# Down projection of 18 half experts in seven block products instead of eight, in a kernel of retention and two mixture-of-experts layers

## The reference

```python
# layer 1: N, D, E, F = 1536, 512, 8, 1024; layer 2: the same with E = 4
for e in range(E):
    h = np.maximum(x @ w1[e], 0.0)        # [1536, 1024]
    ye = h @ w2[e]                        # [1536, 512]
    out += P[:, e:e + 1] * ye
```

## Time and profile before

| | us |
|---|---|
| median of 3 runs | 1545.9 (1545.72 to 1546.02) |
| profiled execution, first to last instruction (span) | 1544.1 |
| profiled execution, own time | not listed apart from the span |
| TensorE busy | 1538.1 (100%) |
| VectorE busy | 880.1 (57%) |
| ScalarE busy | 446.9 (29%) |
| GpSimd busy | 49.5 (3%) |

### The profile page before, as it was taken

The page is one execution under the profiler, slowest core; times in us unless marked ns, Lnnn a source line. Parts: engine busy times, 40 slices in busy tenths (PEclk is TensorE's granted clock), DMA queues, the critical chain, the costliest instruction groups (busy, mean ns, idle before and its releaser), DMA issues.

```text
span 1544.1 us, 21412 instructions
## 1 busy us (share of the span) xinstructions
PE 1538.1 (100%) x8306; PEld 1396.6 (90%) x8306; DVE 880.1 (57%) x1419; ACT 446.9 (29%) x865; POOL 49.5 (3%) x45
## 2 busy tenths in 40 slices
PE   9999999999999999999999999999999999999999
PEld 8999989998999899989998999899998999899988
DVE  7756855555546455555565555576555556555553
ACT  5432322331223213222232132243331223213311
POOL 6100000000000000000000000012000000000000
PEclk9999999999999999999999999999999999999999
DMA  9100101101001011010010110101101001011011
GB/s 347 56 28 28 55 1 55 55 1 56 28 27 54 0 54 54 0 54 27 27 54 0 54 54 2 55 1 55 55 1 55 28 28 54 0 54 55 1 44 66
DMA packets 34458, 66.56 MB, mean 43 GB/s; under 512 B 2016, under 2 KB 2528, under 8 KB 34400
## 3 DMA queue, kind: packets, MB, share of 16 engines
q1 hardware_dynamic: 34256, 65.65, 12.3%
q10 hardware_dynamic: 144, 0.10, 0.0%
HBM read 62.59 MB, written 3.15 MB: 43 GB/s over the span
## 4 chain that ended last, share of the span: by engine, by line
PE 98%; DMA 1%; issue 0%; POOL 0%; SPq 0%; DVE 0%; POOLq 0%
PE banks L1220 17%; PE banks L1221 17%; PE banks L1219 17%; PE banks L1195 15%; PE banks L1199 15%; PE banks L1197 15%; DMA qt_in<-in_q_t 1%; PE banks L1159 0%; PE banks L1105 0%; DMA k_in<-in_k 0%; PE banks L1061 0%; POOL q_up L400 0%; PE banks L1079 0%; PE banks L1141 0%; PE banks L1139 0%
## 5 line engine op out<-in xcount | busy, mean ns | idle before, releaser
L1195 PE MATMUL banks<-x_hi,w_hi 128*128 128x384 f32 x1344 | 450.6, 335 | 0.0
L1199 PE MATMUL banks<-x_hi,w_lo 128*128 128x384 f32 x1344 | 450.3, 335 | 0.0
L1197 PE MATMUL banks<-x_lo,w_hi 128*128 128x384 f32 x1344 | 450.0, 335 | 0.0
L1221 PE MATMUL banks<-w_hi,h_lo 128*128 128x512 f32 x1148 | 448.3, 391 | 0.0
L1220 PE MATMUL banks<-w_lo,h_hi 128*128 128x512 f32 x1148 | 448.2, 390 | 0.0
L1219 PE MATMUL banks<-w_hi,h_hi 128*128 128x512 f32 x1148 | 447.6, 390 | 0.0
L917 DVE SCALAR_TENSOR_TENSOR acc<-banks,gate,acc 128x512 f32<-128x512 f32 x251 | 188.5, 751 | 372.5 <-PE banks L1221 372.5
L591 ACT COPY ups<-banks 128x384 f32<-128x384 f32 x288 | 138.0, 479 | 887.8 <-PE banks L1199 887.8
L869 DVE TENSOR_TENSOR ups<-banks,ups 128x384 f32<-128x384 f32 x288 | 155.6, 555 | 189.5 <-ACT ups L591 167.8
L1221 PEld LDWEIGHTS banks<-w_hi,h_lo 128*128 128x128 f32 x1148 | 215.6, 188 | 44.7
L1219 PEld LDWEIGHTS banks<-w_hi,h_hi 128*128 128x128 f32 x1148 | 215.8, 188 | 43.4
(11 more groups left out here) (105 smaller groups left out, 479.8 us busy)
## 6 DMA issues: line engine op xcount, KB each, us to landing
w_raw<-in_moe_w SPq DMA_DIRECT2D x46, 1024.0 KB, 5.0
kt_in<-in_k_t SPq DMA_DIRECT2D x12, 256.0 KB, 6.9
qt_in<-in_q_t SPq DMA_DIRECT2D x12, 256.0 KB, 8.3
v_in<-in_v SPq DMA_DIRECT2D x12, 256.0 KB, 8.5
k_in<-in_k SPq DMA_DIRECT2D x10, 256.0 KB, 8.8
out<-acc SPq DMA_DIRECT2D x2, 768.0 KB, 3.5
out<-acc SPq DMA_DIRECT2D x5, 256.0 KB, 2.0
w_raw<-in_moe_w SPq DMA_DIRECT2D x4, 256.0 KB, 9.6
```

The source lines that it names most:

```text
L1195: nc.tensor.matmul(o, w1_hi[:, w, kc, fs], x_hi[:, x, kc, at], start=start and kc == 0, stop=False, skip_group_check=True)
L1197: nc.tensor.matmul(o, w1_hi[:, w, kc, fs], x_lo[:, x, kc, at], start=False, stop=False, skip_group_check=True)
L1199: last = nc.tensor.matmul(o, w1_lo[:, w, kc, fs], x_hi[:, x, kc, at], start=False, stop=kc == 1, skip_group_check=True)
L1221: last = nc.tensor.matmul(o, h_lo[:, f, b, rows], w2_hi[:, f, :], start=False, stop=(n == UC - 1))
```

## The change

Eighteen of the 24 units become "fast": units 3 to 14 of layer 1 and 17 to 22 of layer 2 (`FAST_1 = 3`, `FAST_2 = 17`, `N_FAST = 18`). Units 0 to 2, 15, 16 and 23 keep the old code. In a fast unit:

- **Down products.** The hidden block matrix (2 token halves by 2 feature halves) times `w2` (2 feature halves by 2 output halves) is done in seven products, each with three token tiles, two feature tiles and three matmuls of 256 columns: 18 matmuls to a product, 126 to a pair, in place of 72 of 512 columns. They are accumulated on PSUM banks 2 to 7, which the up products share.
- **Hidden blocks.** Besides the three sums of the up projection, VectorE forms four sums of hidden blocks (`s1` to `s4`) and seven low parts, ScalarE the seven high parts, all in instructions of 128x768 instead of 128x384.
- **Adding to `acc`.** The batch 0 rows are added by VectorE in two steps to a tile (`add_wy`, `add_u3`). The batch 1 rows are multiplied by the gate and written to `stage1` and `stage2` by ScalarE (nine small instructions to a pair), and GpSimd adds these to `acc` with two accumulating DMAs of 768 KB to a pair. The stages lie in the memory of the first four blocks of `h_hi`, so the next pair's `a11_high` waits for the first DMA and its `s_high` of block S1 for the second.
- **Weights.** The sums of `w1` and the four new sums of `w2` move to (or are made on) GpSimd, eight subtractions or additions of 128x512 to a unit. `w2` is now seven blocks to split; the high parts are ScalarE's. The up products run in another order: `W_A12` and `W_A22` ahead of `W_S4`.
- The DMA scratch in SBUF is set to 1024 bytes.

```diff
+FAST_PRODUCTS = [
+    (W_A11, X_B11, ON_X, True), (W_S2, X_T2, ON_X, False), (W_S3, X_T3, ON_Y, True), (W_S1, X_T1, ON_X, False),
+    (W_A12, X_B21, ON_Z, True), (W_A22, X_T4, ON_Y, False), (W_S4, X_B22, ON_X, False),
+]
+DOWN_PRODUCTS = [(H_A11, V_B11), (H_A22, V_T4), (H_A12, V_B21), (H_S1, V_T1), (H_S2, V_T2), (H_S3, V_T3), (H_S4, V_B22)]
+D_P1, D_P4, D_P2, D_P5, D_P6, D_P7, D_P3 = range(7)
...
             # TensorE
+            def fast_up(k, f, p):
+                n = PAIRS * f + p
...
+                    if w == W_S3 and layer_starts: ...
+                    elif w == W_S3:
+                        pe.wait_ge(u3_added, CPB * n)
+                        pe.wait_ge(last_staged, CPB * n)
+                    if w == W_S1:
+                        pe.wait_ge(u2_copied, n + 1)
+                    if w == W_A22:
+                        pe.wait_ge(h_summed, 3 * n + 1)
...
+            def fast_down_proj(f, p):
+                for product, (h, v) in enumerate(DOWN_PRODUCTS):
+                    pe.wait_ge(fast_h_lo[h], n + 1)
...
+                    for t in range(CPB):
...
+                        if product == D_P6:
+                            pe.wait_ge(p1_staged, CPB * n + (t + 1))
+                        elif product == D_P7:
+                            pe.wait_ge(u2_staged, CPB * n + (t + 1))
+                        elif product == D_P3:
+                            pe.wait_ge(wy_added, CPB * n + (t + 1))
+                        o, rows = down_psum(product, t), slice(t * P, (t + 1) * P)
+                        for kc in range(2):
+                            nc.tensor.matmul(o, h_hi[:, h, kc, rows], w2_hi[:, v, kc, :], ...)
+                            nc.tensor.matmul(o, h_hi[:, h, kc, rows], w2_lo[:, v, kc, :], ...)
+                            last = nc.tensor.matmul(o, h_lo[:, h, kc, rows], w2_hi[:, v, kc, :], ...)
...
             # GpSimd, one fast unit
+            def add_stage1(f, p):
+                pool.wait_ge(p1_staged, CPB * n + CPB)
+                pool.wait_ge(u2_staged, CPB * n + CPB)
+                pool.dma_start(rows, stage1, accum_op=ALU.add).then_inc(stage1_added, 16)
+            def add_stage2(f, p):
+                pool.wait_ge(stage1_added, 16 * n + 16)
+                pool.wait_ge(last_staged, CPB * n + CPB)
+                pool.dma_start(rows, stage2, accum_op=ALU.add).then_inc(stage2_added, 16)
+            def fast_unit(f):
+                for n in range(4):
+                    w2_sum_of(f, n)
+                if f not in (0, N_FAST_1):
+                    add_stage2(f - 1, 1)
+                add_stage1(f, 0)
+                w1_sum_of(f, 0)
+                w1_sum_of(f, 1)
+                add_stage2(f, 0)
+                w1_sum_of(f, 2)
+                w1_sum_of(f, 3)
+                add_stage1(f, 1)
...
             # ScalarE, pair 0 of a fast unit
+                copy_p1(k, 0, 0); copy_p1(k, 0, 1); gate_column(gate, col); copy_u2(k, 0)
+                t23_high(f); t41_high(f); copy_u4(k, 0, 0); b11_high(k, f); copy_u4(k, 0, 1); b2_high(k, f)
+                a11_high(f, 0); a22_high(f, 0); a21_relu(f, 0); a12_high(k, 0)
+                s_high(f, 0, H_S1); stage_p1(f, 0, 0); s_high(f, 0, H_S2); stage_p1(f, 0, 1)
+                s_high(f, 0, H_S3); s_high(f, 0, H_S4); stage_p1(f, 0, 2)
+                stage_u2(f, 0, 0); stage_u2(f, 0, 1); stage_u2(f, 0, 2)
+                stage_last(f, 0, 0); stage_last(f, 0, 1); copy_p1(k, 1, 0); stage_last(f, 0, 2); copy_p1(k, 1, 1)
...
             # VectorE, pair 0 of a fast unit
+                t23_low(f); t41_low(f); sum22(k, f, 0); b11_low(f); sum11(k, f, 0)
+                relu_low(f, 0, H_A11, ...); sum21(k, f, 0); b2_low(f); relu_low(f, 0, H_A22, ...)
+                s1(f, 0); relu_low(f, 0, H_A12, x_pair); s2(f, 0); s_low(f, 0, H_S1); s3(f, 0); s4(f, 0)
+                s_low(f, 0, H_S2); s_low(f, 0, H_S3); add_wy(f, 0, 0, ...); add_wy(f, 0, 1, ...)
+                s_low(f, 0, H_S4); add_wy(f, 0, 2, ...); add_u3(f, 0, 0, ...); add_u3(f, 0, 1, ...); add_u3(f, 0, 2, ...)
...
-                nc.vector.tensor_copy(w2_hi[:, at, :], raw[:, at, :]).then_inc(w2_hi_ready, 1)    # in fast units: ScalarE
...
-    nc = _bacc.Bacc("TRN2", target_bir_lowering=False, num_devices=1)
+    nc = _bacc.Bacc("TRN2", target_bir_lowering=False, num_devices=1, dynamic_dma_scratch_size=1024)
```

More of the change, by code:

```diff
@@ L333, in _, with w1_split @@
             sp.dma_start(gate2[:, :, :], moe2_probs.rearrange("p (i e) -> p i e", e=E2)).then_inc(gate2_in, 16)
[L335 to L346, removed]
+            def w1_split(k, f=None):
+                if f is None:
+                    sp.wait_ge(w1_ready, w1_before(k) + 4)
+                else:
+                    for m in (W_A11, W_S1, W_A12, W_A22):
+                        sp.wait_ge(fast_w1_lo[m], f)
+                    sp.wait_ge(fast_w1_summed, 4 * f)
@@ new lines, in fast_unit @@
+            def fast_unit(k, f, gate, col):
+                if not is_first(f):
+                    act.wait_ge(last_staged, PAIRS * CPB * f)
+                copy_p1(k, 0, 0)
+                copy_p1(k, 0, 1)
+                gate_column(gate, col)
+                copy_u2(k, 0)
+                t23_high(f)
+                t41_high(f)
+                copy_u4(k, 0, 0)
+                b11_high(k, f)
+                copy_u4(k, 0, 1)
+                b2_high(k, f)
+                a11_high(f, 0)
+                a22_high(f, 0)
+                a21_relu(f, 0)
+                a12_high(k, 0)
+                s_high(f, 0, H_S1)
+                stage_p1(f, 0, 0)
+                s_high(f, 0, H_S2)
+                stage_p1(f, 0, 1)
+                s_high(f, 0, H_S3)
+                s_high(f, 0, H_S4)
+                stage_p1(f, 0, 2)
+                stage_u2(f, 0, 0)
+                stage_u2(f, 0, 1)
+                stage_u2(f, 0, 2)
+                stage_last(f, 0, 0)
+                stage_last(f, 0, 1)
+                copy_p1(k, 1, 0)
+                stage_last(f, 0, 2)
+                copy_p1(k, 1, 1)
+                copy_u2(k, 1)
+                w1_high(k, f, W_A11)
+                copy_u4(k, 1, 0)
+                copy_u4(k, 1, 1)
+                w1_high(k, f, W_S1)
+                w1_high(k, f, W_A12)
+                a11_high(f, 1)
+                w1_high(k, f, W_S3)
+                a22_high(f, 1)
+                w1_high(k, f, W_A22)
+                a21_relu(f, 1)
+                w1_high(k, f, W_S2)
+                a12_high(k, 1)
+                s_high(f, 1, H_S1)
+                s_high(f, 1, H_S2)
+                stage_p1(f, 1, 0)
+                stage_p1(f, 1, 1)
+                w1_high(k, f, W_S4)
+                s_high(f, 1, H_S3)
+                stage_p1(f, 1, 2)
+                s_high(f, 1, H_S4)
+                stage_u2(f, 1, 0)
+                stage_u2(f, 1, 1)
+                stage_u2(f, 1, 2)
+                stage_last(f, 1, 0)
+                stage_last(f, 1, 1)
+                stage_last(f, 1, 2)
@@ L931, in down, with sum22 @@
                         split_w1_low(k + 1, u)
-            def unit(k, gate, col, how="add"):
-                split_w2(k)
-                hidden(k, 0)
-                down(k, 0, gate, col, how)
-                w1_sums(k + 1)
-                hidden(k, 1)
-                down(k, 1, gate, col, how, split_next=True)
+            def sum22(k, f, p):
+                dve.wait_ge(u4_copied, 2 * (PAIRS * f + p) + 2)
+                dve.wait_ge(up_done, ups_before(k, p) + (2 * UP_AT[W_S3] + 2))
+                raw = h_raw[:, R_A11, :, :]
+                nc.vector.tensor_tensor(raw, y_pair, raw, ALU.add).then_inc(h_summed, 1)
```

653 lines of the change are left out of this document (564 added, 89 removed).

## The result

| | before | after |
|---|---|---|
| median, us | 1545.8 (1545.71 to 1546.02, 4 runs) | 1511.9 (1511.85 to 1512.66, 4 runs) |
| ratio | | 0.9782 (0.9768 to 0.9796) |
| span of the profiled execution, us | 1544.1 | 1510.2 |

The account below looks back on a forecast made before the run. TensorE was taken as the bound, matmuls times their step. Span 1544.1 - 46.4 (gain) + 2 (`sum22`) + 3 (first fast units) + 1 (leaving them) = 1503.7, plus 1.8 to the median: 1505.5 us, range 1498 to 1535.

Parts of the forecast that it names:

- Gain on TensorE: Down products in the fast pairs: 126 matmuls at 119.6 ns replace 16.36 us by 15.07, saving 1.29 us a pair, 46.4 us.
- Fit: Claim that VectorE (44.7 us a unit), ScalarE (about 35) and GpSimd (10.2) still fit in the 59.3 us available.
- `sum22`: VectorE's sum that `W_A22` waits for in each pair: 0.25 us left for the semaphore, 0.05 a pair taken, 2 us.
- The first fast units: First fast unit of each layer: late `w2` load and GpSimd sums make `W_A22` 1.6 us late, twice, 3 us.
- `D_P6` with 0.7 us of slack: Down product S2 times T2, at 23.2 us of a pair; its low part is ready at 22.5, costing nothing.
- The accumulating DMA: GpSimd's two DMAs a pair: issue to landing, D, taken as 8 us between 3.5 and 12.6, and so hidden.
- free up to D = 11: With D us from a DMA's issue to landing, no cost up to 11; each us beyond costs 2 us a pair.
- Leaving the fast units: After a layer's last fast pair, ScalarE's relu waits for the second DMA: nothing to 2 us, 1 taken for both.
- rival 3: Chain and DMA cost just eat the gain: 1.2 to 1.4 us a pair, 1543 to 1549 us; chance 0.03.
- rival 2: VectorE chain longer than added up, still faster: 1516 us from hand-overs, 1535 with GpSimd overlaps; chance 0.22.
- Rivals 1 to 3: The first: landing of the second accumulating DMA becomes the bound, 1614 us at the upper end, chance 0.15.
- the forecast proper: The outcome around the predicted 1505.5 us, 1498 to 1514 us, with chance 0.58.

## Why the prediction was right, and where it was off

- **Gain on TensorE.** Right: 29.68 us a pair against 29.66. The step of 120 ns, read from 23 matmuls at the end, holds in a stream of 126. The three widths of before were enough; 45.7 us were gained. By the formula of the Trainium skill (TensorE: Matmul & The Clock Gate, Back-to-back issue gap) it would have been 64. The forecast called it the gap in a stream; that section gives it for a matmul by itself, and 131 ns at 512 columns for a stream of weight loads and matmuls. The trace has 227 there, so it agrees with neither figure.
- **Fit.** Right: VectorE 22.36 us in the pair above and 21.57 in the next, 43.9 a unit for the 44.7 worked out. Its 768-element instructions are 0.95 us; ScalarE's staged ones are longer than the rows that I took (476 for 376 ns, 687 for 620), which cost nothing.
- **`sum22`.** 2 us taken, nothing lost.
- **The first fast units.** 3 us forecast, 2.7 measured. Moving four sums removes both waits and gives 1.4 to 2.3 us of it.
- **`D_P6` with 0.7 us of slack.** In steady pairs no wait, as forecast. The slack of the stop before it is measured, 1.1 and 1.35 us ("1.0 or more" in the forecast). `D_P6`'s own I only read from the timeline, about 1.0 in pair 0; no run isolates it. The run with the longer chain fits it: 1.98 us more in the chain and TensorE 1.07 late by then take 0.9 of the slack, and `D_P6` starts there 0.06 us behind the end of its low part.
- **The accumulating DMA.** Hidden, as forecast; D is 5.8 to 6.1 us, where I took 8 from bounds of 3.5 and 12.6. The claim "free up to D = 11" is borne out up to 9.2 (18.3 us for the whole chain of three landings, which the forecast counts as 2D), but only with the two sums of `w1` ahead of the DMA and inside the fast units. Beyond it the price is more than 2 us a pair per us: a chain of 24.1 us is D = 12.1, for which the forecast gives 2.1, and 2.9 were measured; one of 26.9 is D = 13.5, forecast 4.9, measured 6.9.
- **Leaving the fast units.** 1 us taken, no wait of TensorE seen. With one DMA more it is the first place to lose time, 11.6 us.
- **The price of rival 3.** Its 1543 to 1549 counts 1.2 to 1.4 us a pair on top of a sum without other losses, 1499.5, where rival 2 counts on 1505.5; from there it is 1549 to 1556.
- **Missed:** the stretch at TensorE's jump back in layer 2. It's the one term that the sum hadn't, 8.7 us, and most of what lies between the 1505.5 predicted and 1511.9. Without it (the run with one unit to a pass, 1502.7) the sum would have been 3 us too high, by the costs taken for `sum22` and for leaving. That 1511.9 still lies inside 1498 to 1535, and inside the 1514 of the forecast proper, is luck as far as this term goes: the room above 1505.5 was made for other losses, which didn't come. Rivals 1 to 3 didn't come about; rival 2's mechanism was near, though: a shift of two sums by 10 us in GpSimd's list is enough for 11 us.

**Open.** Why layer 2's loop loses its code from pass to pass and layer 1's, as long, doesn't. Moving the loop in the code didn't settle it, and that the stretch is a want of code is itself a reading, borne out by the kernels with half the body and with straight code. Nor is shown whether the size of the stretch (4.3 to 7.7 us over four kernels) depends on the DMAs that run beside it.

## What to carry to other kernels

A change that makes a loop body longer in instructions (here 126 matmuls for 72) can have a price at the jump back which no row of before shows (one of the two loops here paid it): keep the body as short as the work allows, and look in the trace after for one long "issue" wait at it. When elementwise work goes to GpSimd, look at what it stands behind in that engine's list: a DMA wait ahead of it decides at what time it runs, and so which VectorE instructions it blocks. Slack is spent once; beyond it a stop costs more than its own length.

## What the runs showed of the hardware that I had not expected

- TensorE stood 4.3 to 7.7 us at one jump back with no other engine late, with its granted clock at 0.50 afterwards.
- A VectorE instruction of 0.68 us with both inputs in SBUF took 2.04 beside two GpSimd sums, one of 0.95 took 2.05 (beside one); one with an input in PSUM kept its 0.94.
- After a wait of 4.7 us TensorE made 8 matmuls of 512 columns in 3 us; after one of 0.8 us the clock stayed at 1.00 and only the next steps were longer (0.22 for 0.12).
- An accumulating DMA of 768 KB from SBUF to SBUF lands in 5.8 us, also when two or three follow each other; its issue is a record of 0.9 us on GpSimd, with the next instruction's start 0.56 us behind its own.
